# Heads of a pair at partitions 0 and 64: each level product of the attention as two 48-row tiles of 64 columns

## The reference, cut to what matters

```python
def _attn_ref(q, k, v, alpha):
    B, H, S, D = q.shape            # 4, 8, 768, 48
    for t in range(S):
        state = alpha[:, :, t, :, None] * state + np.einsum('bhd,bhe->bhde', k[:, :, t], v[:, :, t])
        y[:, :, t] = np.einsum('bhd,bhde->bhe', q[:, :, t], state)
```

## Time and profile before

| | value |
|---|---|
| time, median of 3 runs | 961.2 us (960.73 to 964.46) |
| profiled execution, its span | 960.8 us |
| PE busy / PEld busy | 892.8 us (93%) / 853.9 us (89%) |
| DVE / POOL / ACT busy | 614.1 / 338.0 / 300.5 us |
| level products (L356), matmul records | 1344, 193.6 us busy |

### The profile page before, as it was taken

The page is one execution under the profiler, slowest core; times in us unless marked ns, Lnnn a source line. Parts: engine busy times, 40 slices in busy tenths (PEclk is TensorE's granted clock), DMA queues, the critical chain, the costliest instruction groups (busy, mean ns, idle before and its releaser), DMA issues.

```text
span 960.8 us, 17012 instructions
## 1 busy us (share of the span) xinstructions
PE 892.8 (93%) x5656; PEld 853.9 (89%) x5656; DVE 614.1 (64%) x1094; ACT 300.5 (31%) x658; POOL 338.0 (35%) x505
## 2 busy tenths in 40 slices
PE   6985889899999999899999999899999999998998
PEld 5885778897899999797999989898999999996998
DVE  5778786877648764686748775585847866533132
ACT  2314434432243313423133322523125231431121
POOL 6574553343405352253514443142522534000000
PEclk9967899999999999999999999999999999997999
DMA  6242333202003020301003020110203000000000
GB/s 132 70 91 71 87 85 76 38 1 51 1 16 60 1 51 1 73 6 34 17 1 75 1 50 2 48 31 10 41 2 74 2 13 2 26 1 0 1 25 25
DMA packets 113227, 33.43 MB, mean 35 GB/s; under 512 B 105168, under 2 KB 111184, under 8 KB 113136
## 3 DMA queue, kind: packets, MB, share of 16 engines
q1 hardware_dynamic: 113136, 32.27, 15.1%
HBM read 27.53 MB, written 4.72 MB: 34 GB/s over the span
## 4 chain that ended last, share of the span: by engine, by line
PE 81%; DVE 10%; issue 4%; ACT 2%; POOL 1%; SPq 1%; DMA 0%; DVEq 0%; POOLq 0%; ACTq 0%
PE aps L356 16%; PE hps L412 9%; PE acc L412 9%; PE acc L414 9%; PE acc L413 9%; PE hps L414 9%; PE hps L413 9%; PE aps L379 2%; PE aps L380 2%; DVE in_l L841 2%; PE aps L404 2%; PE hps L493 2%; PE aps L337 2%; DVE Qx L768 2%; PE aps L392 1%
## 5 line engine op out<-in xcount | busy, mean ns | idle before, releaser
L1023 POOL TENSOR_TENSOR K<-K,T 96x192 f32<-96x192 f32 x224 | 163.0, 728 | 209.3 <-PE aps L356 208.5
L356 PE MATMUL aps<-Qx,K 96*128 96x128 f32 x1344 | 193.6, 296 | 23.0 <-DVE Qx L789 15.9
L356 PEld LDWEIGHTS aps<-Qx,K 96*128 96x128 f32 x1344 | 183.1, 207 | 31.2 <-DVE Qx L789 16.8
L789 DVE TENSOR_TENSOR Qx<-Qx,T 96x384 f32<-96x384 f32 x224 | 156.0, 697 | 56.2 <-PE aps L356 51.6
L913 DVE SCALAR_TENSOR_TENSOR hid_l<-hps,hid_h 128x384 fp32r<-128x384 f32 x96 | 53.7, 560 | 132.6 <-ACT hid_h L702 132.4
L796 DVE COPY_PREDICATED Pm<-level_mask,aps 128x384 f32<-128x384 uint8 x160 | 119.4, 747 | 0.0
L702 ACT ACTIVATE hid_h<-hps 128x384 fp32r<-128x384 f32 x96 | 47.2, 492 | 230.5 <-PE hps L414 229.9
L1025 POOL TENSOR_TENSOR T<-T 96x192 f32<-96x192 f32 (+6 forms) x224 | 108.8, 486 | 17.6
L1008 POOL TENSOR_TENSOR Pm<-ident,qk 128x1536 f32<-128x1536 f32 x16 | 44.6, 2790 | 188.4 <-DVE qk L754 188.4
L412 PE MATMUL hps<-in_h,w_h 128*128 128x384 f32 x288 | 102.3, 355 | 0.1
L414 PE MATMUL hps<-in_h,w_l 128*128 128x384 f32 x288 | 98.2, 341 | 0.0
(11 more groups left out here) (108 smaller groups left out, 1654.9 us busy)
## 6 DMA issues: line engine op xcount, KB each, us to landing
a_raw<-in_alpha SPq DMA_DIRECT2D x64, 72.0 KB, 2.3
k_raw<-in_k SPq DMA_DIRECT2D x64, 72.0 KB, 2.3
q_raw<-in_q SPq DMA_DIRECT2D x64, 72.0 KB, 2.3
vx<-in_v SPq DMA_DIRECT2D x64, 72.0 KB, 2.3
out<-x SPq DMA_DIRECT2D x24, 192.0 KB, 1.9
x<-in_moe_w_ch SPq DMA_DIRECT2D x9, 256.0 KB, 2.8
x<-in_moe_w_ch SPq DMA_DIRECT2D x12, 192.0 KB, 2.4
x<-in_moe_w_v SPq DMA_DIRECT2D x8, 192.0 KB, 2.9
```

The costliest lines, as they stand in the source:

```text
L356: mm = pe.matmul(bank(6 + j)[:, c * P:(c + 1) * P], K[:, cc * P:(cc + 1) * P], Qx[0:HP, :, cc * P:(cc + 1) * P].rearrange("p s (n x b) -> ...
L789: nc.vector.tensor_tensor(Qright(l, h), Qright(l, h), t_left, ALU.mult).then_inc(s_Qu, 1)
L1023: nc.gpsimd.tensor_tensor(kl, kl, t_right.unsqueeze(2).to_broadcast([HP, nb, B]), ALU.mult).then_inc(s_Ku, 1)
```

## The change

The heads of a pair now lie on partitions 0 to 47 and 64 to 111 (`HS` = 64, `HR` = 112); the 16 rows between hold zeros (three small memsets of the raw tiles at the start). `Qx` becomes `Q` with one copy. A level product of a chunk becomes two, one for each head, each with 48 rows of K (128 columns, stationary) and 48 rows of Q (64 columns, moving). Head `e` writes to its own bank, `bank(6 + 2 * l + e)`, which holds both pairs, so that the copies out of PSUM now go head by head and wait for both pairs. The products of the first level also wait for K of both pairs. L768 becomes one tensor_tensor, the multiplication of Q works on one copy, and L803 is gone. The transposes and the state work on 112 rows instead of 96.

```diff
@@ tensor
                             if j == 0:
                                 pe.wait_ge(s_T, 2 * U + 2)
-                            elif j > 2:
-                                kept(pe, U, j - 3)
+                                pe.wait_ge(s_K, 2 * U + 2)
+                            elif h == 0:
+                                kept(pe, U, 2 * l - 3)
+                                kept(pe, U, 2 * l - 2)
                             for c in range(HC):
                                 cc = h * HC + c
-                                mm = pe.matmul(
-                                    bank(6 + j)[:, c * P:(c + 1) * P], K[:, cc * P:(cc + 1) * P],
-                                    Qx[0:HP, :, cc * P:(cc + 1) * P].rearrange(
-                                        "p s (n x b) -> p s n x b", x=2, b=1 << l)[:, :, :, 1, :],
-                                    start=True, stop=True)
+                                for e in range(2):
+                                    rows = slice(e * HS, e * HS + D)
+                                    mm = pe.matmul(
+                                        bank(6 + 2 * l + e)[:, cc * HS:(cc + 1) * HS], K[rows, cc * P:(cc + 1) * P],
+                                        right(Q[rows, cc * P:(cc + 1) * P], l), start=True, stop=True)
                             mm.then_inc(s_lv, 1)
...
-                                              K[:, cc * P:(cc + 1) * P], ident[0:HP, 0:HP])
+                                              K[:, cc * P:(cc + 1) * P], ident[0:HR, 0:HR])
...
@@ scalar
-                        for h in range(2) if l >= ML else ():
-                            j = 2 * l + h
-                            act.wait_ge(s_lv, 2 * LV * U + j + 1)
+                        for e in range(2) if l >= ML else ():
+                            act.wait_ge(s_lv, 2 * LV * U + 2 * l + 2)
...
@@ vector
-                        for s in range(2):
-                            ins = nc.vector.scalar_tensor_tensor(
-                                out=Qx[0:HP, s, cols], in0=bank(2)[0:HP, 0:HT], scalar=head_mask[:, s:s + 1],
-                                in1=T[:, cols], op0=ALU.mult, op1=ALU.mult)
+                        ins = nc.vector.tensor_tensor(Q[0:HR, cols], bank(2)[0:HR, 0:HT], T[:, cols], ALU.mult)
                         ins.then_inc(s_Q, 1)
...
-                            t_left = T[:, h * HT + B - 1:(h + 1) * HT:2 * B].unsqueeze(2).unsqueeze(1).to_broadcast([HP, 2, nb, B])
-                            nc.vector.tensor_tensor(Qright(l, h), Qright(l, h), t_left, ALU.mult).then_inc(s_Qu, 1)
-                            if l >= ML:
-                                continue
-                            keep = Pm[:, h * HC:(h + 1) * HC, :, :].rearrange(
-                                "p c s (n x b) -> p (c s) n x b", x=2, b=B)[:, :, :, 1, :]
+                            t_left = T[:, h * HT + B - 1:(h + 1) * HT:2 * B].unsqueeze(2).to_broadcast([HR, nb, B])
+                            q_right = right(Q[0:HR, h * HT:(h + 1) * HT], l)
+                            nc.vector.tensor_tensor(q_right, q_right, t_left, ALU.mult).then_inc(s_Qu, 1)
+                        for e in range(2) if l < ML else ():
+                            keep = Pm[:, :, e, :].rearrange("p c (n x b) -> p c n x b", x=2, b=B)[:, :, :, 1, :]
...
-                    for h in range(2):
-                        dve.wait_ge(s_Qu, 2 * LV * (U + 1) - 1 + h)
-                        cols = slice(h * HT, (h + 1) * HT)
-                        nc.vector.tensor_tensor(Qx[0:HP, 0, cols], Qx[0:HP, 0, cols], Qx[0:HP, 1, cols],
-                                                ALU.add).then_inc(s_Qc, 1)
```

More of the change, by code:

```diff
@@ L42, in build @@
     HP = 2 * D
+    HS = 64
+    HR = HS + D
     NP = NH // 2
@@ L78, in build @@
         level_mask = sb("level_mask", [P, P], U8)
[L79 to L84, removed]
+        head_mask = sb("head_mask", [HR, 2])
+        q_raw = sb("q_raw", [P, NC, 2, HS])
+        k_raw = sb("k_raw", [P, NC, 2, HS])
+        a_raw = sb("a_raw", [P, NC, 2, HS])
         vx = sb("vx", [P, NC, 2, HP])
-        Qx = sb("Qx", [P, 2, S])
-        K = sb("K", [HP, S])
-        T = sb("T", [HP, S])
+        Q = sb("Q", [P, S])
+        K = sb("K", [HR, S])
+        T = sb("T", [HR, S])
         Pm = sb("Pm", [P, NC, 2, P])
         qk = sb("qk", [P, NC * 2])
-        carry = sb("carry", [HP, NP, HP])
-        k_tok = sb("k_tok", [P, NC, HP])
+        carry = sb("carry", [HR, NP, HP])
+        k_tok = sb("k_tok", [P, NC, HR])
         state = K[:, 0:NC * HP].rearrange("p (c d) -> p c d", c=NC)
-        qk_prod = k_tok[:].rearrange("p c d -> p (c d)")
+        qk_prod = k_tok[:].rearrange("p c d -> p (c d)")[:, 0:NC * HP].rearrange("p (c d) -> p c d", d=D)
         xT = sb("xT", [P, KT, HT + 1])
@@ L204, in left, with right, raw_rows @@
             return ap.rearrange("p (n x b) -> p n x b", x=2, b=1 << l)[:, :, 0, :]
-        def Qright(l, h):
-            return Qx[0:HP, :, h * HT:(h + 1) * HT].rearrange(
-                "p s (n x b) -> p s n x b", x=2, b=1 << l)[:, :, :, 1, :]
+        def right(ap, l):
+            return ap.rearrange("p (n x b) -> p n x b", x=2, b=1 << l)[:, :, 1, :]
+        def raw_rows(raw, c):
+            return raw[:, c, :, :].rearrange("p e d -> p (e d)")[:, 0:HR]
         def kept(eng, U, j):
@@ L391, in attention @@
                             both = both.rearrange("p (g x) -> p g x", x=D)[:, 0:4:3, :]
-                            mm = pe.matmul(bank(23 + h)[0:HP, c * HP:(c + 1) * HP], k_tok[:, cc, :],
+                            mm = pe.matmul(bank(23 + h)[0:HR, c * HP:(c + 1) * HP], k_tok[:, cc, :],
                                            both, start=True, stop=True)
@@ L404, in attention @@
                             mm = pe.matmul(y_bank[h][0:HP, c * P:(c + 1) * P], before,
-                                           Qx[0:HP, 0, cc * P:(cc + 1) * P], start=False,
+                                           Q[0:HR, cc * P:(cc + 1) * P], start=False,
                                            stop=(c == HC - 1))
@@ L590, in attention @@
                             act.wait_ge(s_turn, 6 * U + 3 * h + i + 1)
-                            nc.scalar.copy(dst[:, h * HT:(h + 1) * HT], bank(i)[0:HP, 0:HT]).then_inc(s, 1)
+                            nc.scalar.copy(dst[:, h * HT:(h + 1) * HT], bank(i)[0:HR, 0:HT]).then_inc(s, 1)
                     yield
@@ L940, in _ @@
             splits = weights()
+            for raw in (a_raw, k_raw, q_raw):
+                nc.vector.memset(raw[:, :, 0, D:HS], 0.0).then_inc(s_zero, 1)
             nc.vector.memset(vx[:], 0.0).then_inc(s_zero, 1)
```

46 lines of the change are left out of this document (23 added, 23 removed).

## The result

| | before | after |
|---|---|---|
| time, median of 4 runs each | 962.57 us (960.73 to 964.46) | 1011.64 us (1006.97 to 1018.59) |
| profiled execution, its span | 960.8 us | 1005.2 us |

The ratio is 1.053 (95% interval 1.0471 to 1.0589): slower by 49 us. The forecast was 1059 us, so the direction and the range held and the size was 47 us too high. The profiled execution of after took 1006.97 us, the shortest of its four; the traces therefore show 44.4 us of the 49.

What follows compares the result with a forecast made beforehand. The prediction took TensorE, busy for 93% of the span, as the bound: 960.8 + 69 (loads) + 30 (switch) + 3 (112 rows) - 4 (VectorE) = 1058.8 us by profiled span, forecast 1059 us, range 946 to 1137.

Steps and rivals of the forecast that it cites:

- What bounds the kernel: TensorE busy 93% of the span; in the dense stretch work added to it lengthens the span nearly one for one.
- Loads, +69 us: Level products: doubled weight loads overlap only partly, adding 0.62 us to each of 112 levels, 69 us; chance 0.33.
- load A2 starts at 0.11, ... load B1 right behind it: Order within a chunk (A, B heads; 1, 2 passes): B1 loads only after matmul A2 leaves at 0.165, giving 0.33 us.
- loads of the two heads always overlap, with the switch paid: Rival: loads for separate rows in level products always overlap, but tile switches still cost 30 us; 980 us, chance 0.20.
- bounds 147 us apart: Limits for the level products' loads: +143 us if none overlap, -4 us if the two heads' loads always overlap.
- The sign that the prediction named for being wrong: A level's group of products staying at or under 1.36 us, or dense matmuls changing their 0.17 us.
- Switch of tiles, +30 us: TensorE drains between tile shapes: 0.15 us in, 0.19 out, together 0.35 for each of 86 stretches of level products.
- 112 rows, +3 us: Transposes of K move and state products load 112 columns instead of 96: 1 us and 2 us more.
- VectorE, -4 us: VectorE's saved work, hidden behind TensorE, and its new order taken together: 4 us gained.
- The relief: At most 114 of VectorE's 614 us go, mostly hidden; between 0 and 18 us gained.
- the order: On VectorE head 0's copy stands behind both multiplications of Q; the next level's wait replaces today's 0.55 to 0.72 us.

Runs made afterwards that it cites:

- Heads apart: The changed kernel with the loops over chunk and head exchanged, three chunks of head 0 and then three of head 1: 1052.67 us, 1.093 of before.
- the isolated pair: Two kernels, each the kernel before plus one unused 64-column product per level, on 48 rows (1016.96 us) or on 96 rows (981.49 us).
- four banks: The changed kernel with level products of the first two units rotating over four banks instead of three: 996.2 us, 1.0404 of before.

## Why the prediction was right or wrong

**What bounds the kernel: right.** TensorE is idle in the dense part as much as before, and each tenth of a microsecond added to a level lengthened the span.

**Loads, +69 us: wrong, and the largest error.** The step that failed is "by these rows load A2 starts at 0.11, ... load B1 right behind it". It took the order in which instructions leave as the order in which loads start. The runs showed that load B1 starts together with A1, and matmul B1 with matmul A1, ahead of load A2: the pair costs what one load did. Measured in the steady level the term is about 0 (24 products in 1.24 us behind the first, 11 of the old in 1.25). The rival "loads of the two heads always overlap, with the switch paid" held. The Trainium skill, TensorE: Matmul & The Clock Gate, The mechanism, says that a load for row groups without conflict is pulled ahead; the traces agree (1.42 us for 24 loads on separate rows, 2.82 on the same), and the matmuls went with their loads. I gave this rival 0.20 because no row of before had such loads. The step also treated bounds 147 us apart as if their middle were likeliest, when each end was a mechanism and the middle needed a third. Heads apart is where something in between does appear, by another way: head 1 starts three pairs late. The sign that the prediction named for being wrong, a group at or under 1.36 us, was not set well either: full overlap gave 1.49, because the way in adds 0.14 to each group whatever the loads do.

**Switch of tiles, +30 us: right.** In 0.14 and out 0.20 us, against 0.15 and 0.19 worked out from the 32-column products; 0.32 us by the isolated pair, some 27 us over the 86 stretches. The Trainium skill, TensorEngine Tiling (Array Packing), Key Properties, says that a change of the mode drains TensorE. The traces agree with a cost at each change, now for 64-row tiles too, and with all 112 rows it is gone.

**112 rows, +3 us: right in kind.** State products stand 0.098 us apart instead of 0.085, transposes of K 0.096 instead of 0.082 (medians): 160 and 80 of them, 3 us.

**VectorE, -4 us: the mechanism was named, sign and size were wrong.** The text says that the first pair waits for the copy of head 0 "some 0.35 + 0.75 us after TensorE's last product" and then sets it equal to the wait it replaces. The relief and the order do not offset each other. The relief (82 us of VectorE's time) shortened nothing that can be found; it was not tried by itself. The order costs 5 us alone and, with the shared bank, 12.5 us in the head; at the doubled levels clock drops add some 6 us (12.1 against 6.5, one profile each). Some +18 stands where -4 was forecast, an error of 22 us in the other direction than that of the loads.

**How much was luck.** The two errors, 69 us too much and 22 too little, leave the 47 us by which the forecast was off. Most of the forecast rise was for a cost that is not there, and without the second error the forecast would have been 69 us too high. That the time rose was right for a reason that the prediction had, the switch; the range held because it was drawn around every rival.

**The ledger** of the 44.4 us between the traces: head 16.2 = 12.5 for the bank + 3.7 that are left, for switches and wider products; dense part 31.6 = 26.0 for these (0.31 us a stretch) + 5.6 that are left, for the doubled levels; tail -3.3, where before ran 7.5 us at 1.2 GHz and after did not. The sum of 980 us for the rival that held, with +30 and +3 as they were and the order's cost put at some +18 instead of a gain, gives 1008; the median is 1012.

**What was not tried.** Both row tiles of a pair of products writing to one bank, which would free the rotation without a fourth bank; no run here shows whether two tiles that run side by side may do that.

## What to carry to other kernels

Splitting a product with a masked operand into row tiles halves the moving columns, but when the weight loads were as long as the matmuls it gained nothing here: overlapping loads only pay back the loads that the split added. Each stretch of tiled products between full ones then cost some 0.32 us, so short stretches woven into dense work are the worst place for it. When buffers rotate, check which buffer of the step before each part needs after a regrouping; and when a rival is a mechanism with a rule behind it, do not take a point between the bounds that has none.

## What the runs showed of the hardware

- Loads for rows 0 to 47 and 64 to 111 start within a hundredth of a microsecond of each other and share 0.11 us, and so do their matmuls (47.27 and 47.28 with four banks). On the same rows, with 48, 96 or 112 of them, loads stand in line at 0.11.
- With six pairs of load and matmul of one head ahead of those of the other, the second head starts 0.28 us late, past three pairs that wait: 1.76 us a group, 1.49 alternating.
- Going from tiles of 128 rows to tiles of 48 and back costs 0.14 us on the way in and 0.20 on the way out; with 96 or 112 rows there is no such cost.
- At 1.2 GHz a group is 2.83 us instead of 1.56, and the six idle stretches of 1 us at the doubled levels were each followed, some 2 us later, by some 3 us at 1.2 GHz in after. TensorE had been busy between. The row for 11.50 to 34.00 in the earlier trace rows reads 1.00, while products ran at half pace there (12 records in 3.07 us): the pace of products is the surer sign.
